# Attention and mixture of experts: VectorE's block of ranks and gates split over two steps, its one-hot tables three to a step, and one filling product at the head

## Chip, cores and metric

The kernel runs on one core of a Trainium2 chip. The metric is the device time of one execution in microseconds (us), the median of several runs. The core has five engines with an instruction queue each: TensorE (matrix products, PE in the rows), VectorE (DVE), ScalarE (ACT), GpSimd (POOL) and SyncE (SP, which issues most transfers). An engine takes its instructions in order and waits on semaphores.

## What is computed

Causal attention over a window of 128 with a distance bias, and then a layer that sends each token to one of eight experts, each of which takes at most `capacity` tokens in the order of their numbers:

```python
scores = scale * np.matmul(q, k.transpose(0, 1, 3, 2))      # (4, 8, 576, 64) each
mask = (rel >= 0) & (rel < window)                           # window = 128
scores = np.where(mask, scores + bias[None], -1000000000.0)
attn = np.exp(scores - scores.max()); attn /= attn.sum() + 1e-09
x = np.matmul(attn, v)                                       # to (2304, 512)
logits = x @ w_gate                                          # 8 experts
expert_idx = np.argmax(logits, axis=1)
# token i goes to slot counts[e] of its expert e while that is below capacity
h = np.maximum(np.einsum('ecd,edf->ecf', disp, w1), 0.0)
y = np.einsum('ecf,efd->ecd', h, w2)
out[i] = gate_w[i] * y[expert_idx[i], pos[i]]                # gate_w: its softmax probability
```

## The kernel before

**Passes and steps.** Four batches are worked in two passes (`batch(0)`, `batch(1)`), two batches in each. A pass has 9 tiles of 128 tokens, and each tile two steps, one for four of the eight heads. So a pass has 18 steps, `kk` 0 to 17; below, "step n" is step n of the second pass. All engines have a function `batch` that runs over the same steps, and semaphores tie them together.

**TensorE in a step:** transposes of the next q tile (even steps) or k tile (odd steps) by `turn` (L1280); of the probabilities of this step (L1322); `turn_back` (L1352), which brings the result of the step before back to token order with its logits, and which waits for `biased`, the count of minima, since it writes the PSUM bank in which the scores of the next step lay; the scores of the step after next (L1314); and `mix` (L1341), probabilities times values, first with the tile's own values and then with `v_step` and the part of the probabilities that GpSimd has masked.

**VectorE in a step:** in odd steps the copy of the turned k (`turned_k`, L930) and the inverse of the sums (`invert_sums`, L936 and L938); `normalise` of the step before (L949, L955, and in even steps the logits' reduce L961); `pick` (L907) and `bias_minimum` (L920) for the step after next; and behind these the work on routing, when it is due.

**ScalarE in a step:** copies out of PSUM and the exponentials of the next step, which wait for the minima. **GpSimd in a step:** `keep_later` (L624), a mask over the probabilities, in odd steps `step_v` (L605), and its share of the routing's tables, `place_in_columns` (L630).

**Routing** is done in three groups of tiles: group 0 is the nine of the first pass, group 1 the next five, group 2 the last four. For group 0 in the steps 1 to 8 and for group 1 in the steps 10 to 17 (in the code `since` counts from the group's first step, 0 and 9) VectorE finds the expert (`find_top`, `find_best`, since 1), its one-hot row (`choose`, since 2), and at since 4 takes the ranks that TensorE has counted and runs `rank_and_weigh`: the gate and, for each token, `key` (its column of slots) and `within` (its place in the column). From these, tables are made: `in_tile` by VectorE (L1023) and `in_column` by GpSimd (L630), one of each for a tile of tokens. TensorE multiplies the two to find out which token fills which slot. For group 0 it does so at step 10 for expert 0's first tile, for the rest behind the steps.

**The head.** TensorE starts with transposes of the identity (`fill_early`, L1457) that nobody reads, and turns the first q and the first k tile between them. Their rows come by four transfers, issued by SyncE (L444) and ScalarE (L801) for half a tile each.

Of the kernel before, what the change touches and what calls it, by code (L numbers as in the profile page):

```python
# [34 lines left out]
def attention_moe(nc, q, k, v, w_gate, w1, w2, capacity, out):  # L35
# [54 lines left out]
    with ctx:  # L90
# [433 lines left out]
        def _(pool):  # L524
# [102 lines left out]
            def place_in_columns(n, lo, hi):  # L627
                pool.wait_ge(keys_ready, n + 1)
                for u in range(lo, hi):
                    g.tensor_scalar(in_column[:, u, :], iota_key[:, :], key[:, u:u + 1], None,  # L630
                                    ALU.is_equal).then_inc(onehots_ready, 1)
# [10 lines left out]
            for b in range(SPANS):  # L642
                for kk in range(STEPS):
                    u = b * TI + kk // 2
                    if kk >= 2:
                        keep_later(b, kk)
                    if b == 1 and kk == FIRST_INVERTED + 1:
                        gather_first()
                    if kk % 2 == 1 and u + 1 < UNITS and (u + 1) % TI > 0:
                        step_v(u + 1)  # L650
                    if 0 <= b * STEPS + kk - 4 < 4 * CHUNKS:
                        split_weights(b * STEPS + kk - 4)
                    if b == 1 and 5 <= kk < FIRST_ROUTED[1]:
                        place_in_columns(0, 2 * (kk - 5), GROUPS[0][1] if kk == 8 else 2 * (kk - 4))
            place_in_columns(1, *GROUPS[1])
            place_in_columns(2, BY_DVE, UNITS)

# [232 lines left out]
        def _(dve):  # L890
# [3 lines left out]
            def link(ins):  # L894

                steps[0] += 1
                ins.then_inc(dve_step, 1)
                dve.wait_ge(dve_step, steps[0])
# [85 lines left out]
            def choose(lo, hi):  # L984

                vec.tensor_tensor(onehot[:, lo:hi, :], by_expert(iota_e[:, :], lo, hi),
                                  by_token(best[:, lo:hi], E), ALU.is_equal).then_inc(onehot_ready, 1)
                vec.tensor_tensor(less_top[:, lo:hi, :], logits[:, lo:hi, :], by_token(top[:, lo:hi], E),
                                  ALU.subtract).then_inc(less_ready, 1)
# [6 lines left out]
                                         .rearrange("p (u e) -> p u e", e=E),  # L996
                                         onehot[:, lo:hi, :], ALU.mult)

            def rank_and_weigh(n, lo, hi):

                if n == 2:
                    own_ranks(n, lo, hi)
                dve.wait_ge(expd_ready, n + 1)
                link(vec.tensor_reduce(gate_sum[:, lo:hi], expd[:, lo:hi, :], AX.X, ALU.add))
                vec.tensor_reduce(rank[:, lo:hi], own_rank[:, lo:hi, :], AX.X, ALU.add)
                link(vec.tensor_scalar(gate_eps[:, lo:hi], gate_sum[:, lo:hi], 1e-9, None, ALU.add))

                vec.tensor_scalar(rounded[:, lo:hi], rank[:, lo:hi], -(P - 1) / 2, ROUND_TO_128, ALU.add, ALU.add)  # L1010
                link(vec.reciprocal(gate[:, lo:hi], gate_eps[:, lo:hi]))
                dve.sem_inc(gate_ready, 1)
                link(vec.tensor_scalar(past[:, lo:hi], rounded[:, lo:hi], ROUND_TO_128, None, ALU.subtract))
                vec.scalar_tensor_tensor(out=key[:, lo:hi], in0=best[:, lo:hi], scalar=float(P * KEEPS),
                                         in1=past[:, lo:hi], op0=ALU.mult, op1=ALU.add)
                link(vec.tensor_tensor(within[:, lo:hi], rank[:, lo:hi], past[:, lo:hi], ALU.subtract))
                dve.sem_inc(keys_ready, 1)

            def place_in_tiles(lo, hi):
                for u in range(lo, hi):  # L1020
                    if EARLY <= u < BY_DVE:
                        vec.tensor_scalar(in_column[:, u, :], iota_key[:, :], key[:, u:u + 1], None, ALU.is_equal)
                    vec.tensor_scalar(in_tile[:, u, :], iota_p[:, :], within[:, u:u + 1], mark[:, u:u + 1],  # L1023
                                      ALU.is_equal, ALU.mult).then_inc(tiles_placed, 1)

            def batch(b, first=False, last=False):
                for kk in range(STEPS):
# [53 lines left out]
                                          cap[:, 0:1], None, ALU.is_lt)  # L1081
                    if last and since == 4:
                        dve.wait_ge(early_kept, 1 if n == 0 else 3)
                        rank_and_weigh(n, lo, hi)
                    if last and n == 1 and since == 5:
                        vec.tensor_copy(is_full_i[:, :], is_full[:, :]).then_inc(is_full_ready, 1)
                    if last and since >= 5:
                        at = lo + (2 * (since - 5) if n == 0 else max(0, 2 * since - 11))
                        place_in_tiles(at, hi if n == 0 and since == 8 else
                                       min(hi, at + (1 if n == 1 and since == 5 else 2)))  # L1090

            vec.memset(v_front[0:HALF, :], 0.0).then_inc(v_front_zeroed, 1)
            link(vec.memset(eps[:, :], 1e-9))
# [32 lines left out]
            find_top(*GROUPS[2])  # L1126
            find_best(*GROUPS[2])
            choose(*GROUPS[2])
            rank_and_weigh(2, *GROUPS[2])
            place_in_tiles(*GROUPS[2])  # L1130

# [142 lines left out]
        def _(pe):  # L1274
# [183 lines left out]

            fill_early(16)
            turn_q(0, 0)  # L1460
            fill_early(4)
            turn_k(0, 0, probsT_ps)
            fill_early(4)
            score(0, 0)
# [191 lines left out]
```

## Time and profile before

| | before |
|---|---|
| time, median of 3 runs (lowest to highest) | 392.94 us (392.62 to 393.62) |
| the profiled execution: its time, its span | 392.7 us, 390.9 us |
| TensorE busy | 375.1 us (96%) |
| VectorE, ScalarE, GpSimd busy | 252.2, 202.0, 144.5 us |
| first pass, second pass, then the experts (from the span's start) | to about 69, 135, 385 us |

The span runs from the first to the last recorded instruction of one execution. "Busy" is time with an instruction under way. TensorE's matmuls overlap, so its share tells little of how near it is to its peak; what costs time are its idle stretches, and what they wait for. In a timeline an instruction's own time is given as well as the idle time ahead of it.

### The profile page before, as it was taken

Reading aid. Unit: us, or ns where it says so; the run is one execution under the profiler, and the core shown is the slowest. Engines: PE = TensorE matmul, PEld = TensorE weight load, DVE = VectorE, ACT = ScalarE, POOL = GpSimd, SP = SyncE. Lnnn points to the kernel's source line nnn. Section 1 sums busy time; section 2 is a strip of 40 time slices with the busy share of each in tenths; the row PEclk is TensorE's granted clock in tenths of the full one; section 3 lists DMA queues with packets and bytes.
Section 4 is the critical chain, followed back from the end, with each engine's and each line's share of the span. In section 5 each row is a group of like instructions: output and inputs, shape, how many; then the busy total and the mean of one; then the engine's idle time right before and its main releaser. Section 6 shows DMA issues by size and latency. Waiting matters only on the chain.

```text
span 390.9 us, 8488 instructions
## 1 busy us (share of the span) xinstructions
PE 375.1 (96%) x2978; PEld 324.2 (83%) x2978; DVE 252.2 (65%) x797; ACT 202.0 (52%) x535; POOL 144.5 (37%) x192
## 2 busy tenths in 40 slices
PE   7999999998999999999999999999999999999990
PEld 7787788786877677989999989889899899989980
DVE  6788677799988673867966546556768674441120
ACT  2978878886887613645634424534646544311100
POOL 7548989935742542232050023034051340020011
PEclk9999999999999999999999999999999999999997
DMA  8999999999751112877685365554787664010001
GB/s 167 201 308 196 231 235 223 263 262 212 169 107 42 43 29 73 268 242 229 200 283 169 119 226 167 179 185 159 238 271 225 195 214 154 3 47 25 2 21 55
DMA packets 81324, 64.87 MB, mean 166 GB/s; under 512 B 63982, under 2 KB 63982, under 8 KB 81264
## 3 DMA queue, kind: packets, MB, share of 16 engines
q1 hardware_dynamic: 73600, 52.19, 49.9%
q0 software_dynamic: 3840, 11.03, 8.6%
q10 hardware_dynamic: 3824, 0.80, 1.1%
q8 instruction: 44, 0.72, 0.8%
q14 instruction: 16, 0.13, 0.1%
HBM read 54.56 MB, written 11.02 MB: 168 GB/s over the span
## 4 chain that ended last, share of the span: by engine, by line
PE 79%; POOL 10%; DVE 5%; issue 2%; ACT 1%; DVEq 0%; POOLq 0%
PE ps L1483 59%; PE ps L1341 4%; PE ps L1314 4%; POOL weights_sb L617 4%; PE ps L1280 3%; PE ps L1352 3%; PE ps L1476 2%; POOL probsT L624 2%; PE ps L1322 2%; POOL v_step L605 2%; POOL weights_sb L616 2%; PE ps L1457 1%; DVE ps L907 1%; DVE probs L920 1%; PE ps L1398 0%
## 5 line engine op out<-in xcount | busy, mean ns | idle before, releaser
L1483 PE MATMUL ps<-rowsT_hi,weights_sb 128*128 128x256 f32 (+2 forms) x512 | 118.2, 309 | 0.9 <-DVE rowsT_lo L1161 0.9
L1483 PE MATMUL ps<-weights_sb,hiddenT 128*128 128x512 f32 x480 | 118.3, 393 | 0.0
L1483 PEld LDWEIGHTS ps<-weights_sb,hiddenT 128*128 128x128 f32 x480 | 88.0, 188 | 16.4 <-DVE hiddenT L1180 0.2
L857 ACT ACTIVATE hiddenT<-ps 128x384 fp32r<-128x384 f32 (+1 forms) x64 | 30.6, 478 | 115.9 <-PE ps L1483 102.6
L1483 PEld LDWEIGHTS ps<-rowsT_hi,weights_sb 128*128 128x128 f32 x512 | 87.0, 188 | 2.5 <-issue 1.4
L1188 DVE TENSOR_TENSOR weights_sb<-raw,weights_sb 128x1024 fp32r<-128x1024 f32 x56 | 68.5, 1223 | 17.7 <-ACT weights_sb L845 15.6
L1483 PE MATMUL ps<-rowsT_lo,weights_sb 128*128 128x256 f32 (+2 forms) x256 | 78.2, 306 | 0.0
L1180 DVE SCALAR_TENSOR_TENSOR hiddenT<-ps,hiddenT 128x384 fp32r<-128x384 f32 (+1 forms) x64 | 34.5, 540 | 59.4 <-ACT hiddenT L857 57.3
L845 ACT ACTIVATE weights_sb<-raw 128x1024 fp32r<-128x1024 f32 x56 | 58.9, 1052 | 0.0
L682 POOL DMA_INDIRECT gathered<-x_rows,src_row x21 | 22.0, 1049 | 92.8 <-DVE weight_now L1174 88.2
L743 ACT ACTIVATE probs<-probs,mins 128x128 f32<-128x128 f32 x144 | 55.7, 393 | 0.4 <-DVE mins L920 0.4
L696 POOL DMA_INDIRECT out<-y_sb,dst_row x21 | 24.4, 1160 | 84.0 <-DVE y_sb L1194 80.3
L1483 PEld LDWEIGHTS ps<-rowsT_lo,weights_sb 128*128 128x128 f32 x256 | 48.2, 188 | 1.2
L624 POOL TENSOR_SCALAR_AFFINE_SELECT probsT<-probsT 128x512 f32<-128x512 f32 x32 | 20.3, 635 | 42.0 <-ACT probsT L769 42.0
L1314 PE MATMUL ps<-kT,qT 64*64 64x192 f32 (+3 forms) x480 | 28.8, 333 | 0.0
L743 ACT ACTIVATION_READ_ACCUMULATOR probs<-probs,mins 128x1 f32 x144 | 27.7, 192 | 0.0
L769 ACT ACTIVATE probsT<-ps 128x512 f32<-128x512 f32 x36 | 21.4, 595 | 10.3 <-PE ps L1322 10.2
L1352 PE MATMUL ps<-eye_wg,mixT 128*128 128x144 f32 x144 | 24.2, 291 | 2.5 <-DVE mins L920 2.5
L949 DVE TENSOR_TENSOR x_sb<-ps,inv_sums 128x256 f32<-128x256 f32 x36 | 15.3, 424 | 15.6 <-PE ps L1352 14.9
L1194 DVE TENSOR_SCALAR y_sb<-ps,weight_now 128x512 f32<-128x512 f32 x23 | 16.1, 747 | 13.9 <-PE ps L1483 13.9
L907 DVE COPY_PREDICATED ps<-later,ps 128x256 f32<-128x256 int32 (+1 forms) x64 | 22.1, 391 | 4.6 <-PE ps L1314 4.5
L1341 PE MATMUL ps<-probsT,v_rows 128*64 128x128 f32 x288 | 23.7, 285 | 0.1
(174 smaller groups left out, 491.6 us busy)
## 6 DMA issues: line engine op xcount, KB each, us to landing
raw<-in_moe_w SPq DMA_DIRECT2D x64, 512.0 KB, 5.1
q_rows<-in_q SPq DMA_DIRECT2D x16, 256.0 KB, 5.9
v_rows<-in_v SPq DMA_DIRECT2D x16, 256.0 KB, 5.7
x_rows<-x_sb SPq DMA_DIRECT2D x16, 256.0 KB, 4.9
k_rows<-in_k SPq DMA_DIRECT2D x14, 256.0 KB, 6.2
k_rows<-in_k ACTq DMA_DIRECT2D x2, 256.0 KB, 6.8
v_rows<-in_v SPq DMA_DIRECT2D x4, 128.0 KB, 5.6
v_front<-in_v SPq DMA_DIRECT2D x4, 128.0 KB, 6.2
```

The costliest lines, as they stand in the source:

```text
L624: g.affine_select(out=probsT[:, 1, :, :], in_=probsT[:, 0, :, :], compare_op=ALU.is_gt, fill=0.0, base=0, pattern=[[0, QUAD], [-1, P]], ch ...
L696: g.indirect_dma_start(out, bass.IndirectOffsetOnAxis(ap=rows[:, i:i + 1], axis=0), y_sb[:, i, :], None, bounds_check=N - 1, oob_is_err=Fa ...
L743: last = nc.scalar.activation(pr, pr, ACT.Exp, bias=mins[:, kk % 2, n:n + 1], scale=-1.0, accum_out=sums[:, i, h:h + 1])
L845: nc.scalar.activation(weights_sb[:, parity(e), 2 * layer, RAW * j:RAW * (j + 1)], raw[:, j, :], ACT.Copy).then_inc(w_hi[layer], 1)
L857: nc.scalar.activation(hiddenT[0][c % RINGED][:, 0:P * size], hiddenT_ps(c, P * size), ACT.Relu).then_inc(hiddenT_hi, 1)
L907: vec.copy_predicated(both[:, :, 2 * P - earlier[i]:2 * P], later[:, own].bitcast(I32).unsqueeze(1).broadcast_to([P, 2, earlier[i]]), both ...
L1180: vec.scalar_tensor_tensor(out=hiddenT[1][c % RINGED][:, 0:P * size], in0=hiddenT_ps(c, P * size), scalar=0.0, in1=hiddenT[0][c % RINGED][ ...
L1188: vec.tensor_tensor(weights_sb[:, parity(e), 2 * layer + 1, part], raw[:, j, :], weights_sb[:, parity(e), 2 * layer, part].bitcast(F32), A ...
L1314: ins = te.matmul(scores_ps(kk % 2, odd)[rows, 2 * P * n + first:2 * P * n + last], qT[part, u % 2, h // 2, rows], keys, start=True, stop= ...
L1341: last = te.matmul(mixT_ps[DH * odd:DH * odd + DH, n, :], left[:, DH * h:DH * h + DH], probsT[:, part, 2 * odd + n, :], start=(part == 0), ...
L1352: last = te.matmul(back_ps(kk % 2)[:, c, :], mixT[:, c, :], eye_wg[:, 2 * quad + c, :], start=True, stop=True)
L1483: ins = te.matmul(dst, left[a], right[c], start=first and n == 0, stop=last and n == 2)
```

## The change

At since 4 VectorE runs only the first half of the block, now `sum_ranks` (the sums of the gate and of the ranks, with `rounded`). The second half, still `rank_and_weigh` (the reciprocal, `past`, `key`, `within`), runs at since 5, behind that step's minima. The tables follow from since 6. For group 0 they are three in each of the steps 6, 7, 8, where two stood in 5, 6, 7 and three in 8, on VectorE and GpSimd alike. For group 1 they are one, two, two in the steps 15, 16, 17, where they stood in 14, 15, 16. Group 2 runs both halves one behind the other as before. At the head one transpose of the identity stands between the first q and the first k tile, not four.

```diff
@@ -650,8 +650,8 @@
                         step_v(u + 1)
                     if 0 <= b * STEPS + kk - 4 < 4 * CHUNKS:
                         split_weights(b * STEPS + kk - 4)
-                    if b == 1 and 5 <= kk < FIRST_ROUTED[1]:
-                        place_in_columns(0, 2 * (kk - 5), GROUPS[0][1] if kk == 8 else 2 * (kk - 4))
+                    if b == 1 and 6 <= kk < FIRST_ROUTED[1]:
+                        place_in_columns(0, 3 * (kk - 6), 3 * (kk - 5))
             place_in_columns(1, *GROUPS[1])
             place_in_columns(2, BY_DVE, UNITS)
 
@@ -996,9 +996,7 @@
                                          .rearrange("p (u e) -> p u e", e=E),
                                          onehot[:, lo:hi, :], ALU.mult)
 
-            def rank_and_weigh(n, lo, hi):
-
-
+            def sum_ranks(n, lo, hi):
 
                 if n == 2:
                     own_ranks(n, lo, hi)
@@ -1008,6 +1006,9 @@
                 link(vec.tensor_scalar(gate_eps[:, lo:hi], gate_sum[:, lo:hi], 1e-9, None, ALU.add))
 
                 vec.tensor_scalar(rounded[:, lo:hi], rank[:, lo:hi], -(P - 1) / 2, ROUND_TO_128, ALU.add, ALU.add)
+
+            def rank_and_weigh(n, lo, hi):
+
                 link(vec.reciprocal(gate[:, lo:hi], gate_eps[:, lo:hi]))
                 dve.sem_inc(gate_ready, 1)
                 link(vec.tensor_scalar(past[:, lo:hi], rounded[:, lo:hi], ROUND_TO_128, None, ALU.subtract))
@@ -1081,13 +1082,15 @@
                                           cap[:, 0:1], None, ALU.is_lt)
                     if last and since == 4:
                         dve.wait_ge(early_kept, 1 if n == 0 else 3)
+                        sum_ranks(n, lo, hi)
+                    if last and since == 5:
                         rank_and_weigh(n, lo, hi)
                     if last and n == 1 and since == 5:
                         vec.tensor_copy(is_full_i[:, :], is_full[:, :]).then_inc(is_full_ready, 1)
-                    if last and since >= 5:
-                        at = lo + (2 * (since - 5) if n == 0 else max(0, 2 * since - 11))
-                        place_in_tiles(at, hi if n == 0 and since == 8 else
-                                       min(hi, at + (1 if n == 1 and since == 5 else 2)))
+                    if last and since >= 6:
+                        each = 3 if n == 0 else 2
+                        at = lo + max(0, each * (since - 6) - (n == 1))
+                        place_in_tiles(at, lo + each * (since - 5) - (n == 1))
 
             vec.memset(v_front[0:HALF, :], 0.0).then_inc(v_front_zeroed, 1)
             link(vec.memset(eps[:, :], 1e-9))
@@ -1126,6 +1129,7 @@
             find_top(*GROUPS[2])
             find_best(*GROUPS[2])
             choose(*GROUPS[2])
+            sum_ranks(2, *GROUPS[2])
             rank_and_weigh(2, *GROUPS[2])
             place_in_tiles(*GROUPS[2])
 
@@ -1458,7 +1462,7 @@
 
             fill_early(16)
             turn_q(0, 0)
-            fill_early(4)
+            fill_early(1)
             turn_k(0, 0, probsT_ps)
             fill_early(4)
             score(0, 0)
```

The same on VectorE's queue, where a row is an instruction or several alike, with the tiles that it writes and reads. In step 4, behind the minima of step 6, there stood before:

```order
L1006 TENSOR_REDUCE gate_sum<-expd 128x9
L1007 TENSOR_REDUCE rank<-own_rank 128x9
L1008 TENSOR_SCALAR gate_eps<-gate_sum 128x9
L1010 TENSOR_SCALAR rounded<-rank 128x9
L1011 RECIPROCAL gate<-gate_eps 128x9
L1013 TENSOR_SCALAR past<-rounded 128x9
L1014 SCALAR_TENSOR_TENSOR key<-best,past 128x9
L1016 TENSOR_TENSOR within<-rank,past 128x9
L930 COPY kT<-ps 128x4x128
L936 TENSOR_TENSOR sums_eps<-sums,eps 128x8
```

The last two rows belong to step 5. At the same place the changed kernel has:

```order
L1004 TENSOR_REDUCE gate_sum<-expd 128x9
L1005 TENSOR_REDUCE rank<-own_rank 128x9
L1006 TENSOR_SCALAR gate_eps<-gate_sum 128x9
L1008 TENSOR_SCALAR rounded<-rank 128x9
L930 COPY kT<-ps 128x4x128
L936 TENSOR_TENSOR sums_eps<-sums,eps 128x8
```

and at the end of its step 5, where two tables (`in_tile`) stood before:

```order
L1012 RECIPROCAL gate<-gate_eps 128x9
L1014 TENSOR_SCALAR past<-rounded 128x9
L1015 SCALAR_TENSOR_TENSOR key<-best,past 128x9
L1017 TENSOR_TENSOR within<-rank,past 128x9
L949 TENSOR_TENSOR x_sb<-ps,inv_sums 128x256
L955 TENSOR_TENSOR gate_part<-ps,inv_sums 128x32
```

Four small instructions have moved behind the minima of step 7, ahead of step 6's `normalise`. For group 1 the block of step 13 stood ahead of the lower half of the first expert tile's rows (`first_rowsT_lo`) and of step 14:

```order
L1010 TENSOR_SCALAR rounded<-rank 128x5
L1011 RECIPROCAL gate<-gate_eps 128x5
L1013 TENSOR_SCALAR past<-rounded 128x5
L1014 SCALAR_TENSOR_TENSOR key<-best,past 128x5
L1016 TENSOR_TENSOR within<-rank,past 128x5
L1038 TENSOR_TENSOR first_rowsT_lo<-ps,first_rowsT_hi 128x512
L949 TENSOR_TENSOR x_sb<-ps,inv_sums 128x256
```

In the changed kernel its second half stands at the end of step 14, with the flag's copy, ahead of the odd step 15:

```order
L1012 RECIPROCAL gate<-gate_eps 128x5
L1014 TENSOR_SCALAR past<-rounded 128x5
L1015 SCALAR_TENSOR_TENSOR key<-best,past 128x5
L1017 TENSOR_TENSOR within<-rank,past 128x5
L1089 CAST is_full_i<-is_full 128x1
L936 TENSOR_TENSOR sums_eps<-sums,eps 128x8
L938 RECIPROCAL inv_sums<-sums_eps 128x8
L949 TENSOR_TENSOR x_sb<-ps,inv_sums 128x256
```

There the flag's copy and one table stood before, and the four are new.

## Rows read from the trace of the kernel before

**Rows 1.** TensorE's waits, all: who waited for whom, us in total, times, longest.

```profile
PE ps L1352 <- DVE mins L920: 2.5, 3, 1.1
```

**Rows 2.** TensorE's timeline, steps 6 to 8: start, us, instructions, [idle before, releaser].

```profile
92.71 0.66 PE L1280 MATMUL ps<-ident,q_rows 128*128 128x128 f32 x4
...
94.92 0.76 PE L1352 MATMUL ps<-eye_wg,mixT 128*128 128x144 f32 x4 [1.11 <-DVE mins L920]
...
97.44 0.66 PE L1280 MATMUL ps<-ident,k_rows 128*128 128x128 f32 x4
...
100.79 0.66 PE L1280 MATMUL ps<-ident,q_rows 128*128 128x128 f32 x4
...
101.72 0.66 PE L1352 MATMUL ps<-eye_wg,mixT 128*128 128x144 f32 x4
102.30 0.88 PE L1314 MATMUL ps<-kT,qT 64*64 64x128 f32 x16
```

**Rows 3.** VectorE's timeline, steps 4 and 5.

```profile
90.58 0.21 DVE L1011 RECIPROCAL gate<-gate_eps 128x9 f32<-128x9 f32 x1
...
91.15 0.59 DVE L1014 SCALAR_TENSOR_TENSOR key<-best,past 128x9 f32<-128x9 f32 x1
...
91.96 0.69 DVE L930 COPY kT<-ps 128x512 f32<-128x512 f32 x1
92.57 0.41 DVE L936 TENSOR_TENSOR sums_eps<-sums,eps 128x8 f32<-128x8 f32 x1
...
93.70 0.75 DVE L907 COPY_PREDICATED ps<-later,ps 128x256 f32<-128x256 int32 x2
...
95.20 0.67 DVE L1023 TENSOR_SCALAR in_tile<-iota_p,within,mark 128x128 f16<-128x128 f16 x2
```

**Rows 4.** GpSimd's timeline, steps 5 and 6.

```profile
91.09 0.63 POOL L624 TENSOR_SCALAR_AFFINE_SELECT probsT<-probsT 128x512 f32<-128x512 f32 x1 [3.40 <-ACT probsT L769]
91.69 1.28 POOL L605 TENSOR_TENSOR v_step<-v_rows 128x512 f32<-128x512 f32 x1
...
94.56 0.63 POOL L624 TENSOR_SCALAR_AFFINE_SELECT probsT<-probsT 128x512 f32<-128x512 f32 x1 [0.33 <-ACT probsT L769]
```

**Rows 5.** Timelines, steps 14 to 17: ScalarE, VectorE, GpSimd, then TensorE.

```profile
123.46 0.60 ACT L786 ACTIVATE first_rowsT_hi<-ps 128x512 fp32r<-128x512 f32 x1 [0.19 <-PE ps L1419]
...
124.91 0.69 DVE L1038 TENSOR_TENSOR first_rowsT_lo<-ps,first_rowsT_hi 128x512 fp32r<-128x512 f32 x1
...
126.25 0.75 DVE L907 COPY_PREDICATED ps<-later,ps 128x256 f32<-128x256 int32 x2
...
128.08 0.15 DVE L936 TENSOR_TENSOR sums_eps<-sums,eps 128x8 f32<-128x8 f32 x1
...
129.08 0.76 DVE L907 COPY_PREDICATED ps<-later,ps 128x256 f32<-128x256 int32 x2
...
127.48 0.64 POOL L624 TENSOR_SCALAR_AFFINE_SELECT probsT<-probsT 128x512 f32<-128x512 f32 x1 [2.22 <-ACT probsT L769]
128.08 1.29 POOL L605 TENSOR_TENSOR v_step<-v_rows 128x512 f32<-128x512 f32 x1
...
127.46 0.76 PE L1352 MATMUL ps<-eye_wg,mixT 128*128 128x144 f32 x4 [0.68 <-DVE mins L920]
...
130.63 0.73 PE L1352 MATMUL ps<-eye_wg,mixT 128*128 128x144 f32 x4
...
132.71 0.66 PE L1322 MATMUL ps<-ident,probs 128*128 128x128 f32 x4
```

**Rows 6.** The head: weight loads (PEld), issue of k rows, issue to landing.

```profile
5.71 0.87 PEld L1457 LDWEIGHTS ps<-ident 128*128 128x128 f32 x4
6.56 0.77 PEld L1280 LDWEIGHTS ps<-ident,k_rows 128*128 128x128 f32 x4
7.29 0.47 PEld L1457 LDWEIGHTS ps<-ident 128*128 128x128 f32 x4
...
1.70 0.82 SPq L444 DMA_DIRECT2D k_rows<-in_k  x1
...
k_rows<-in_k SPq DMA_DIRECT2D x1, 128.0 KB, 4.8
```

## The prediction, made before the changed kernel had run

> **What bounds the kernel now.** I read the list of waits first, for what TensorE waits for. TensorE is busy 96% of the span, and the largest thing its matmuls wait for is VectorE's minima: three times, 2.5 us [rows 1]. Then TensorE's timeline of the second pass over the batches. A step (two per tile of tokens) begins with the four transposes of L1280. Steps 7 to 8 stand 3.35 us apart (97.44 to 100.79) with TensorE never idle, but step 6 took 4.73 us (92.71 to 97.44) [rows 2]. Its L1352, which starts 0.93 us into a free step (100.79 to 101.72), started 2.21 us in, 1.11 us of it idle for VectorE; restart included the step lost 1.38 us. L1352 waits because it writes the PSUM bank whose scores VectorE must have taken for the next step.
>
> Then VectorE's timeline, for why it was late: after the minima of step 6 it ran the block of ranks and gates to the end (the reciprocal of L1011 at 90.58, next step's copy at 91.96) [rows 3]. And GpSimd's beside it, which shows a second thing. VectorE's key (L1014, 128x9) took 0.59 us, where a sum of 128x8 takes 0.15 [rows 5], and ended at 91.74, when GpSimd's L624 ended (91.09 + 0.63). Its tiny sum L936 took 0.41 us and ended at 92.98, when GpSimd's L605 ended (91.69 + 1.28) [rows 3, 4]. The reciprocals, reduces and PSUM readers beside such work show no stretch. So a VectorE instruction with both inputs in SBUF waits until the GpSimd instruction under way is over.
>
> For the second group the picture repeats at step 15: L1352 at 127.46 after 0.68 us idle [rows 5]. The third stall (step 12) follows code that the change leaves alone. After the attention TensorE runs the experts with no wait on a transfer, so a shift of the attention's end should reach the end of the program whole.
>
> **The change part by part.** Of the eight instructions of the block, four now follow the minima of step 4 (13), and four (reciprocal, past, key, within) those of step 5 (14).
>
> *Group 0, the gain.* Step 5 on VectorE starts where the reciprocal stood, 90.6 instead of 91.96. Its copy takes 0.61 (92.57 less 91.96) [rows 3], so L936 comes at 91.2, into L624 of GpSimd, and ends with it at 91.74. From there the old spacing holds (L936's end 92.98 to L907 93.70, 0.7): L907 at 92.44. TensorE could go 1.22 after L907 (94.92 less 93.70), so at 93.66. Step 6 of TensorE starts at 92.71 as before and its L1352 wants 93.64. The stall is all but gone, and step 7 starts near 96.1 (92.71 plus 3.35) instead of 97.44: 1.3 us won.
>
> *Group 0, what is late next.* The four moved instructions start 1.50 after L907 (93.70 to 95.20) [rows 3], at 93.94. Key comes 0.57 later (90.58 to 91.15), at 94.51. GpSimd's L624 of step 6 stands at 94.56, 1.85 after the step's start [rows 2, 4]; both move forward by 0.07 at most, the time for which the step's first transposes had waited for the late copy. It will run from 94.5 to 95.15. Key, or at the latest within behind it, waits for it, and step 6 of VectorE starts at 95.3. Even steps reach L907 0.75 later, as in the other group (124.91 to 126.25, less the 0.60 of L1038 [rows 5]; the logits' reduce is in it): 96.05; the minimum that TensorE wants at 97.27, against 97.03: 0.24 lost, with the restart 0.34. Then three tables of L1023. Two took 0.67 beside GpSimd's columns [rows 3]; three should take 0.7 to 0.9, from 97.55 to 98.25 or 98.45. The copy puts L936 of step 7 at 98.86 or later. GpSimd's L624 of step 7 is 97.95 to 98.58, and behind it comes L605 with 1.28 us, to 99.86. L936 falls into L605 and waits 1.0 us for its end. L907 then stands at 100.55, the minimum at 101.77; step 8 began at 99.8 and wants it at 100.72. TensorE stalls 1.05, starts L1352 at 101.77 and step 9 2.52 later (94.92 to 97.44) [rows 2]: 104.29. The old step 9 began at 100.79 + 3.35 = 104.14. Group 0 in sum: 0.15 us lost.
>
> At this place a page of the skill bears on the sum. The Trainium skill, SBUF — State Buffer, section "SBUF: two separate sides", says that VectorE and GpSimd share a port pair as an exclusive lock held for a whole instruction, also for a VectorE instruction with two SBUF inputs against a GpSimd one that reads SBUF. The trace agrees (0.59 and 0.41 us, both ending with GpSimd's). By the lock the group loses 0.15 us; by free ports it would win 1.3.
>
> *GpSimd's own queue.* Its columns come three to a step from step 6 instead of two from step 5. They wait for the keys, ready at 95.3 now, and should be through by about 97.2, before L624 of step 7. In step 7 the third one puts L624 of step 8 at about 101.7, some 0.1 late, under TensorE's stall. Nil.
>
> *Group 1, the gain.* L1038 stood at 124.91 behind the block. It needs ScalarE's upper half, ready at 124.06 (123.46 + 0.60) [rows 5], so 124.10 now, and L907 at 125.44 instead of 126.25. The minimum is there at 126.65; TensorE's L1352 wanted 126.78 (127.46 less the 0.68 idle). Stall gone, 0.7 won and 0.1 of restart.
>
> *Group 1, what is late next.* The moved four start at 126.94, key at 127.5 (0.57 behind, as in group 0), within just after. GpSimd's L624 starts at 127.48 [rows 5] and does not move, since the transposes ahead of it don't. Within waits to 128.11, and behind it the flag's copy puts L936 near 128.4. In the old kernel L936 came at 128.08, in the very moment in which L605 started, and passed (0.15 us). Now it waits for L605's end at 129.37 (128.08 + 1.29). L907 of step 15 then comes at 130.1 instead of 129.08, the minimum at 131.3. TensorE's L1352 of step 16 started at 130.63 in the old kernel and would now at 131.3: 0.7 late. Behind it the old step waited for GpSimd before its second half (L1352 to the next L1322, 130.63 to 132.71, is 2.08) [rows 5]; that wait is over by then, so the step, which has no scores, needs only 2.52 less their 0.88 [rows 2], 1.65, and ends near 133.0: 0.3 us lost.
>
> *The head.* Three transposes of the identity go, 0.87/4 = 0.22 us each [rows 6], on paper 0.65 us. But the k rows that follow were issued at 1.70 and landed 4.8 later, at 6.5, and TensorE began to load them at 6.56. The fillers merely covered this transfer. The gain lies between 0 and 0.06; I take 0.
>
> *Sum.* 0.15 + 0.3 + 0 = 0.45 us slower: 392.7 of the profiled execution (span 390.9 and 1.8 around it) becomes 393.15. Its own time lies 0.24 under the median of three, 392.94, which would become 393.4. I say 393.3. This kernel's runs spread by 0.3%, 1.2 us, and less can't be told from no change.
>
> **The rivals.** *The two stalls simply go* (faster). For it: the block is plainly what TensorE waited for. Against it: rows 3 and 4, where L936 and key end with GpSimd's instruction. Needed is that key, within and both L936 miss GpSimd's work, or that the lock is no rule. Then group 0 wins 1.3, group 1 some 0.7 (the minimum of step 16 at 130.0, then held by the exponentials), in all about 2.0: 391.0. Chance 0.20.
>
> *One group escapes* (within the noise). Margins are 0 to 0.3 us: key and within at 94.5 to 94.6 against 94.5, L936 at 98.86 against 98.58, key and within at 127.5 to 127.6 against 127.48. If the first or second is off, group 0 wins 1.0 and the sum is -0.7; if the third, group 1 wins 0.6 and the sum is -0.45: 392.3. Chance 0.18.
>
> *The fast clock comes late* (slower). Four transposes took 0.87 us at 5.71 and 0.47 at 7.29 [rows 6]: TensorE went from 1.2 to 2.4 GHz near 7.1, after fillers and q transposes without a break. Now it idles for 0.6 us (5.93 to 6.56) just ahead of that. If the rise comes only after another stretch of work, the k transposes, the first scores and the q transposes run at the low level, three pieces of 0.4 us each (0.87 less 0.47): 1.2 us, and with the 0.45 a time of 394.5. It decides only if it puts the first exponentials back, since they lead on to the GpSimd chain of the first pass. Chance 0.10. The Trainium skill, TensorE: Matmul & The Clock Gate, Part 4, says that transposes don't count as activity for this gate; that would take the risk away, but the trace, whose transposes sped up after nothing but transposes, speaks against it.
>
> **How the numbers follow.** Forecast (both groups caught by GpSimd) 0.50, own range 392.8 to 393.8; both stalls gone 0.20; one escape 0.18; late clock 0.10; the rest 0.02. The range leaves out the farther half of the fast case and most of the slow one: 391.1 to 394.2. Faster by over 0.3% (under 391.8): 0.22. Slower by over 0.3% (over 394.1): 0.09. Between: 0.69.
>
> **What the profile after would show.** Right: TensorE's stall in step 6 nearly gone, a new one of about 1 us in step 8 behind L936 stretched to about 1 us beside L605; none in step 15, but a late L1352 in step 16, with L936 of step 15 stretched likewise; key or within ending with a GpSimd L624; L1280 of the k rows still at 6.5 to 6.6. Wrong: L936 of 0.16 us in steps 7 and 15, step 9 starting near 103.1, or transposes of 0.22 us after 7.5.

## The result, and the profile after

The changed kernel took 394.46 us (median of 5 runs, 394.16 to 395.5) where the kernel before took 392.89 in the same five turns: ratio 1.0039, 95% interval 1.0024 to 1.0054, so 0.9 to 2.1 us slower. Run again later beside its variants it took 393.98 against 393.06 (1.0021, 1.0011 to 1.0031). Forecast were 393.3, so 0.45 us slower by its sum, and a range to 394.2: the sign of the point was right, its size was two to three and a half times too small (0.45 against 0.92 and 1.57), and the range was too short on that side for the first comparison, while the second one's median lies inside it. One execution each of two kernels below, e5 and e7, took 930 and 2049 us; without it their medians would be 390.66 and 393.31 instead of 390.72 and 393.38.

TensorE's waits after, from the list of waits (who waited for whom, us in total, times, longest), which answer to [rows 1]:

```profile
PE ps L1356 <- DVE mins L920: 2.3, 2, 1.4
PE ps L1284 <- DMA k_rows<-in_k: 1.4, 1, 1.4
PE ps L1284 <- DVE kT L930: 0.6, 1, 0.6
PE ps L1345 <- DVE first_slot L1053: 0.5, 1, 0.5
```

The minima cost TensorE nearly what they did, but in other steps: the sum moved from 2.5 to 2.3 us and a wait for VectorE's copy of kT, which the kernel before did not have, stands beside it. TensorE's timeline of steps 6 to 9 after (start, us, in brackets the idle time ahead), for [rows 2]:

```profile
96.54 0.66 PE L1284 MATMUL ps<-ident,k_rows 128*128 128x128 f32 x4
97.75 0.76 PE L1356 MATMUL ps<-eye_wg,mixT 128*128 128x144 f32 x4
...
100.92 0.66 PE L1284 MATMUL ps<-ident,q_rows 128*128 128x128 f32 x4 [0.57 <-DVE kT L930]
...
102.86 0.76 PE L1356 MATMUL ps<-eye_wg,mixT 128*128 128x144 f32 x4 [0.85 <-DVE mins L920]
...
105.38 0.66 PE L1284 MATMUL ps<-ident,k_rows 128*128 128x128 f32 x4
```

Step 7 began at 96.54 instead of 97.44: the old stall is gone, as forecast. Step 9 began at 105.38 instead of 104.14. From step 5 (89.64 here, 89.29 before) to step 9 TensorE took 15.74 us where it took 14.85. VectorE's and then GpSimd's timeline of the same stretch, for [rows 3, 4]:

```profile
94.86 0.64 DVE L1015 SCALAR_TENSOR_TENSOR key<-best,past 128x9 f32<-128x9 f32 x1
...
96.54 0.75 DVE L907 COPY_PREDICATED ps<-later,ps 128x256 f32<-128x256 int32 x2
98.04 2.22 DVE L1024 TENSOR_SCALAR in_tile<-iota_p,within,mark 128x128 f16<-128x128 f16 x3
100.18 0.68 DVE L930 COPY kT<-ps 128x512 f32<-128x512 f32 x1
100.78 0.15 DVE L936 TENSOR_TENSOR sums_eps<-sums,eps 128x8 f32<-128x8 f32 x1
...
94.85 0.63 POOL L624 TENSOR_SCALAR_AFFINE_SELECT probsT<-probsT 128x512 f32<-128x512 f32 x1 [1.52 <-ACT probsT L769]
...
98.34 0.64 POOL L624 TENSOR_SCALAR_AFFINE_SELECT probsT<-probsT 128x512 f32<-128x512 f32 x1 [0.70 <-ACT probsT L769]
98.94 1.27 POOL L605 TENSOR_TENSOR v_step<-v_rows 128x512 f32<-128x512 f32 x1
```

Read them against each other. Key ends at 95.50, when L624 ends (95.48). The three tables were priced at 0.7 to 0.9 us and took 2.22: they end at 100.26, when L605 ends (100.21). So it is not L936 that waits in step 7 (0.15 us) but the tables ahead of it, and the copy of kT, which would have run beside L605, now stands behind it. That makes the new wait of 0.57 us.

Steps 14 to 17, VectorE, GpSimd and TensorE, for [rows 5]:

```profile
128.72 0.60 DVE L1017 TENSOR_TENSOR within<-rank,past 128x5 f32<-128x5 f32 x1
...
129.53 1.03 DVE L936 TENSOR_TENSOR sums_eps<-sums,eps 128x8 f32<-128x8 f32 x1
...
128.65 0.66 POOL L624 TENSOR_SCALAR_AFFINE_SELECT probsT<-probsT 128x512 f32<-128x512 f32 x1 [2.22 <-ACT probsT L769]
129.28 1.26 POOL L605 TENSOR_TENSOR v_step<-v_rows 128x512 f32<-128x512 f32 x1
...
127.29 0.66 PE L1326 MATMUL ps<-ident,probs 128*128 128x128 f32 x4
127.94 0.73 PE L1356 MATMUL ps<-eye_wg,mixT 128*128 128x144 f32 x4
...
132.49 0.76 PE L1356 MATMUL ps<-eye_wg,mixT 128*128 128x144 f32 x4 [1.41 <-DVE mins L920]
...
136.93 0.73 PE L1487 MATMUL ps<-weights_sb,first_rowsT_hi 128*128 128x512 f32 x2
```

This group went as forecast, each row of it: no wait in step 15, within and L936 both end with a GpSimd instruction, and a late L1356 in step 16. From L1326 of step 15 to the first expert product are 9.64 us, 9.32 before (126.12 to 135.44): 0.32 lost, 0.3 forecast.

Two more differences of this trace were no part of the forecast. Step 5 came 0.35 later: at the head the k rows landed 5.5 us after their issue (4.8 before [rows 6]). And in step 10 TensorE waited 0.54 us for first_slot, the last row of the waits above; this is called the hiccup of step 10 below.

### The profile page after: what moved, and what is told of

Read it like the earlier page. It is cut to its first block, busy times and chain, and to the rows that moved or that the text cites. A ratio compares the mean times of both kernels' runs of the same rounds, so it can differ in the third digit from the quotient of the medians.

```text
span 392.4 us, 8482 instructions
## 1 busy us (share of the span) xinstructions
PE 373.7 (95%) x2975; PEld 322.8 (82%) x2975; DVE 254.4 (65%) x797; ACT 202.0 (51%) x535; POOL 144.6 (37%) x192
## 4 chain that ended last, share of the span: by engine, by line
PE 74%; POOL 10%; DVE 8%; issue 2%; DMA 2%; SPq 1%; ACT 0%; DVEq 0%; POOLq 0%
PE ps L1487 59%; POOL weights_sb L617 4%; PE ps L1345 3%; PE ps L1318 3%; PE ps L1356 3%; PE ps L1480 2%; PE ps L1284 2%; POOL v_step L605 2%; POOL probsT L624 2%; DMA v_rows<-in_v 2%; POOL weights_sb L616 2%; DVE ps L907 2%; PE ps L1326 1%; DVE probs L920 1%; SPq L386 1%
## 5 line engine op out<-in xcount | busy, mean ns | idle before, releaser
L624 POOL TENSOR_SCALAR_AFFINE_SELECT probsT<-probsT 128x512 f32<-128x512 f32 x32 | 20.4, 638 | 42.5 <-ACT probsT L769 40.1
L1356 PE MATMUL ps<-eye_wg,mixT 128*128 128x144 f32 x144 | 24.4, 292 | 2.5 <-DVE mins L920 2.3
L949 DVE TENSOR_TENSOR x_sb<-ps,inv_sums 128x256 f32<-128x256 f32 x36 | 15.2, 424 | 14.7 <-PE ps L1356 13.7
```

The costliest lines, as they stand in the source:

```text
L624: g.affine_select(out=probsT[:, 1, :, :], in_=probsT[:, 0, :, :], compare_op=ALU.is_gt, fill=0.0, base=0, pattern=[[0, QUAD], [-1, P]], ch ...
L1356: last = te.matmul(back_ps(kk % 2)[:, c, :], mixT[:, c, :], eye_wg[:, 2 * quad + c, :], start=True, stop=True)
```

## The experiments

Medians below stand beside those of the kernel before on the same chip. Four kernels shared a chip in each of three batches. Unless said otherwise they have four fillers at the head, so that only the split differs.

**The parts alone.** e1 is the kernel before with one filling product:

```diff
-            fill_early(4)
+            fill_early(1)
             turn_k(0, 0, probsT_ps)
```

> The old kernel with one filling transpose at the head instead of four, nothing else. Theory A (the fillers merely covered the transfer of the k rows; they landed 0.7 us later in the profiled execution of the changed kernel by chance): no change of the time, within 0.3 us of the old kernel, and step 0 of the second pass starts within 0.1 us of the old one's. Theory B (the head is a cause of its own: the transfer lands late whenever the fillers are gone, or the clock comes late): 0.35 us slower or more, with the k transposes near 7.3 again. Theory C (the head was the main part of the loss): over 1 us slower.

e2 is the opposite, the whole change with four fillers.

> The changed kernel with four filling transposes again. Theory A: as slow as the changed kernel but for noise, so about 1.2 to 1.6 us over the old one. Theory B: 1.2 us over the old one (1.55 less 0.35). Theory C: within 0.5 us of the old one.

e3 splits group 0's block alone, with three tables a step there, and e4 group 1's alone. The line that does it in e3 (in e4 it has `(False, True)`; the tables' steps, not shown, follow):

```diff
-                    if last and since == 5:
+                    if last and since == (5 if (True, False)[n] else 4):
                         rank_and_weigh(n, lo, hi)
```

> Only group 0 is changed (its block split over the steps 4 and 5, its tables three to a step on VectorE and GpSimd); group 1 and the head as in the old kernel. Theory A (VectorE's third table and L936 wait for GpSimd's mask and v_step): step 9 starts 0.9 us later than in the old kernel, counted from step 5, and the whole is 0.9 us slower; the three tables of step 6 take some 2.2 us again. Rival (the loss of group 0 in the profiled execution was an accident of its phase, 0.35 us late from the head): 0 to 0.3 us slower, tables of step 6 under 1 us.

> Only group 1 is changed (block split over the steps 13 and 14, tables a step later), the rest as in the old kernel. Theory A: the stall of step 15 gone (0.7 us won), a stall of about 1.4 us in step 16 behind L936 stretched to about 1.0 us, in sum 0.3 us slower. Rival (L936 is on no path that matters, the stall of step 16 comes from group 0's lateness): 0.7 us faster, L936 of step 15 undisturbed.

Measured, with before at 393.11: e1 393.42 (1.0008, 0.9994 to 1.0021), e2 394.28 (1.0024, 1.0011 to 1.0037), e3 394.20 (1.0019, 1.0003 to 1.0035), e4 393.63 (1.0016, 1.0003 to 1.0029). Each half of the split costs something by itself and the head nothing that can be told from nothing. The forecasts for e3 met neither side whole: its tables took 1.07 us, not 2.2 and not under 1, and steps 5 to 9 lost 0.30 us, not 0.9, though its median lies 1.09 over before; the hiccup of step 10 is in its trace and in those of e1 and e2. The medians don't divide 1 us further; the traces do. From step 5 to step 9 TensorE took 14.85 us in e1 and e4, as before, and 15.14 and 15.15 in e2 and e3. From step 15 to the first expert product it took 9.32 in e3, as before, and 9.65 in e2 and e4. So group 0 costs 0.30 here, group 1 costs 0.33, and the two add.

Group 0's loss is 0.30 in these, not the changed kernel's 0.89. Both kernels reach the tables equally far behind the start of step 7, 1.50 and 1.49 us. In e2 VectorE, then GpSimd:

```profile
98.09 1.07 DVE L1024 TENSOR_SCALAR in_tile<-iota_p,within,mark 128x128 f16<-128x128 f16 x3
99.08 0.68 DVE L930 COPY kT<-ps 128x512 f32<-128x512 f32 x1
99.69 0.70 DVE L936 TENSOR_TENSOR sums_eps<-sums,eps 128x8 f32<-128x8 f32 x1
...
98.39 0.72 POOL L624 TENSOR_SCALAR_AFFINE_SELECT probsT<-probsT 128x512 f32<-128x512 f32 x1 [0.70 <-ACT probsT L769]
99.09 1.27 POOL L605 TENSOR_TENSOR v_step<-v_rows 128x512 f32<-128x512 f32 x1
```

Here the tables are done when L605 begins, the copy runs beside L605, and L936 waits for its end (100.39 and 100.36). Which way it goes is decided at L624, as the tables one by one show: the second and the third in the changed kernel, then the same two in e2.

```profile
98.27 0.76 DVE L1024 TENSOR_SCALAR in_tile<-iota_p,within,mark 128x128 f16<-128x128 f16 x1
98.94 1.32 DVE L1024 TENSOR_SCALAR in_tile<-iota_p,within,mark 128x128 f16<-128x128 f16 x1
...
98.32 0.31 DVE L1024 TENSOR_SCALAR in_tile<-iota_p,within,mark 128x128 f16<-128x128 f16 x1
98.54 0.63 DVE L1024 TENSOR_SCALAR in_tile<-iota_p,within,mark 128x128 f16<-128x128 f16 x1
```

In the changed kernel the second table waits for the end of L624, and so the third one meets L605. In e2 the second goes ahead, L624 takes 0.72 us instead of 0.64, and only the third waits for L624. To the nanosecond, L624 starts 70 to 72 ns behind the second table's start in the three traces in which that table waits (the changed kernel, e12 and e7), and 78 to 83 ns behind it in the four in which it doesn't (e2, e3, e8, e11). No row shows more of why.

**Taking the suspect away.** e5 leaves L936 out, so that the reciprocal reads the sums (the 1e-9 is not added), and e6 does the same to the kernel before:

```diff
-                vec.tensor_tensor(sums_eps[:, i, :], sums[:, i, :], eps[:, :], ALU.add).then_inc(sum_step, 1)
-                dve.wait_ge(sum_step, b * 2 * TI + 2 * i + 1)
-                vec.reciprocal(inv_sums[:, i, :], sums_eps[:, i, :]).then_inc(sum_step, 1)
+                vec.reciprocal(inv_sums[:, i, :], sums[:, i, :]).then_inc(sum_step, 1)
```

The later waits on `sum_step`, not shown, are lowered to match.

> The change with four fillers back at the head, and the sum of L936 (the sums of the softmax plus 1e-9, two SBUF inputs of 128x8) left out: the reciprocal reads the sums themselves, so the 1e-9 is not added. Theory (VectorE's instructions with two SBUF inputs, and its f16 tables, wait for the GpSimd instruction under way, and the waits of L936 in steps 5, 7 and 15 are what eats the split's gain): VectorE reaches L907 of step 6 some 0.55 us earlier, key of group 0 misses the GpSimd L624 and takes 0.15 to 0.2 us, steps 5 to 9 of TensorE take 13.4 to 13.7 us where they took 15.14 with the four fillers, the late mixing product of step 16 is on time, and the median is 391.3 to 392.3, 2 to 3 us under the same kernel with the sum. Rival 1 (the wait moves on to the reciprocal or the normalising product behind it): these are stretched to the end of L605 instead, steps 5 to 9 still take over 14.8 us, and the median stays at 394.0 or above. Rival 2 (the price is in the tables alone): step 6's three tables still take over 1 us and catch L605, steps 5 to 9 take about 14.6, the median 393.6.

> The kernel before with the sum of L936 left out in the same way (1e-9 not added), its block of ranks and gates undivided. Control for the run without the sum on the changed kernel: how much of that gain is the shorter VectorE queue alone. Theory: the stall of step 6 shrinks from 1.11 to about 0.5 us (0.41 + 0.25 less on VectorE's queue there), those of steps 12 and 15 (0.67 and 0.68) to 0.2 or less, together 1.4 to 1.8 us: median 391.3 to 391.8, and the split kernel without the sum is then not better by more than 0.5 us. Rival (the lock matters only in the split kernel, where L936 falls into L605): the kernel before gains under 0.6 us, median 392.5 to 393.1, and the split kernel without the sum lies at least 0.8 us below it.

Measured, with before at 392.92: e5 390.72 (0.9942, 0.9928 to 0.9956), e6 392.15 (0.9977, 0.9968 to 0.9985). Without L936 the split kernel is 2.2 us faster than before. The theory's numbers for the steps held; the median fell 0.6 us below its range (391.3 to 392.3). TensorE's timeline in e5:

```profile
92.19 0.66 PE L1282 MATMUL ps<-ident,q_rows 128*128 128x128 f32 x4
93.12 0.66 PE L1354 MATMUL ps<-eye_wg,mixT 128*128 128x144 f32 x4
...
98.89 0.66 PE L1282 MATMUL ps<-ident,q_rows 128*128 128x128 f32 x4
99.82 0.66 PE L1354 MATMUL ps<-eye_wg,mixT 128*128 128x144 f32 x4
102.42 0.66 PE L1282 MATMUL ps<-ident,k_rows 128*128 128x128 f32 x4
```

L1354 stands 0.93 behind each step's start, no wait at all, and steps 5 to 9 take 13.58 us. VectorE in the same trace shows why the gain is more than L936's own duration:

```profile
90.73 0.19 DVE L936 RECIPROCAL inv_sums<-sums 128x8 f32<-128x8 f32 x1
...
93.47 0.17 DVE L1013 SCALAR_TENSOR_TENSOR key<-best,past 128x9 f32<-128x9 f32 x1
...
96.18 0.76 DVE L1022 TENSOR_SCALAR in_tile<-iota_p,within,mark 128x128 f16<-128x128 f16 x3
...
97.45 0.19 DVE L936 RECIPROCAL inv_sums<-sums 128x8 f32<-128x8 f32 x1
```

The reciprocal runs in the middle of L624 (GpSimd has it at 90.63 to 91.27) and is not stretched. So VectorE is early enough for key (0.17 us) and for all three tables (0.76) to be through before the next L624. With the wait of L936 in step 5 went those of key and of the tables behind it, and in step 7 there is no L936 to wait. For e6 the forecast was too good (391.3 to 391.8 against 392.15). The stall of step 6 shrank only to 0.65 us: leaving the sum out saves VectorE 0.45 us there (L936 at 92.57, the reciprocal behind it at 93.02 in the kernel before), not the 0.66 that was put in. That of step 15 stayed (0.68): VectorE's last sum before it is that of step 13, behind which VectorE waits 0.56 us for TensorE's scores, with the sum and without it. The rival for e6 was met in part: the split kernel without the sum lies 1.4 below, where it asked for at least 0.8, but the kernel before gained 0.77, where it allowed under 0.6. That 1.4 us is what the split is worth once L936 is gone.

e8 keeps the sum but gives it one SBUF input:

```diff
-                vec.tensor_tensor(sums_eps[:, i, :], sums[:, i, :], eps[:, :], ALU.add).then_inc(sum_step, 1)
+                vec.tensor_scalar(sums_eps[:, i, :], sums[:, i, :], 1e-9, None, ALU.add).then_inc(sum_step, 1)
```

> The change with four fillers back, and the sum of L936 done by a tensor-scalar instruction (one SBUF input and the constant 1e-9) instead of a tensor-tensor one with two SBUF inputs; same values, same place. Theory A (what makes a small VectorE instruction wait for GpSimd is its second SBUF input): L936 takes 0.15 to 0.2 us in steps 5, 7 and 15 where it took 0.56, 0.70 and about 1, and the kernel gains most of what leaving it out gains: steps 5 to 9 take 13.8 to 14.3 us, median 392.3 to 393.0. Theory B (a tensor-scalar instruction from SBUF to SBUF waits as well, as the f16 tables do): L936 keeps its 0.5 to 1 us, steps 5 to 9 take 15.0 us or more, median 394.0 to 394.4.

Measured: 393.36 (1.0008, 0.9997 to 1.0019), steps 5 to 9 15.15 us. VectorE, steps 5, 7 and 15:

```profile
91.01 0.56 DVE L936 TENSOR_SCALAR sums_eps<-sums 128x8 f32<-128x8 f32 x1
...
99.11 0.70 DVE L936 TENSOR_SCALAR sums_eps<-sums 128x8 f32<-128x8 f32 x1
...
128.48 1.04 DVE L936 TENSOR_SCALAR sums_eps<-sums 128x8 f32<-128x8 f32 x1
```

Theory B: it waits as long with one input as with two. My reading that two SBUF inputs make the wait was too narrow. The median lies between the two theories' ranges, 0.4 over before where e2 and e12 lie 1.2 and 1.3 over; the one trace, equal to e2's in these steps, doesn't show why.

**The tables.** e7 gives step 6 two tables, step 7 three and step 8 four. e9 is e7 without the sum, e10 the changed kernel (one filler, three tables) without the sum.

```diff
-                        each = 3 if n == 0 else 2
-                        at = lo + max(0, each * (since - 6) - (n == 1))
-                        place_in_tiles(at, lo + each * (since - 5) - (n == 1))
+                        tables = ({6: (0, 2), 7: (2, 5), 8: (5, 9)}, {6: (0, 1), 7: (1, 3), 8: (3, 5)})[n].get(since)
+                        if tables:
+                            place_in_tiles(lo + tables[0], lo + tables[1])
```

> The change with four fillers back, its group 0 tables on VectorE two, three and four in steps 6, 7 and 8 instead of three in each. Theory (three tables behind the minima of step 6 end just where GpSimd's L605 begins; a third one that is caught costs 0.6 us more than one that passes): the two take 0.5 to 0.7 us, the copy and L936 of step 7 come 0.4 us earlier but L936 waits for the end of L605 all the same, so that steps 5 to 9 take 14.9 to 15.1 us (15.14 with three tables that passed, 15.74 in the changed kernel, whose third was caught), and the median is 393.8 to 394.1, at most 0.4 us under the run with the four fillers and three tables. Rival (the third table, not L936, is what holds step 8 back): steps 5 to 9 take 14.4 us or less and the median is 393.3 to 393.6.

> A try for the best version: four fillers at the head, the block split in both groups, the sum of L936 left out (1e-9 not added) and group 0's tables two, three and four in steps 6 to 8. Theory (with the sum gone, step 6 to 8 already run without a wait behind VectorE: steps 5 to 9 took 13.58 us, four free steps are 13.4): the distribution of the tables is worth 0.2 us at most now, steps 5 to 9 take 13.4 to 13.6, median 390.5 to 391.0, 1.9 to 2.4 us under the kernel before. Rival (two tables instead of three help by themselves, since a caught table costs 0.6 us in part of the executions): 0.3 us or more under the three tables without the sum, which had 390.72.

> The changed kernel itself, with its one filler, without the sum of L936 (1e-9 not added). Beside the same kernel with four fillers and without the sum (390.72) it prices the head alone, in a kernel that has no other stall left to hide a shift. Theory: the k rows' landing sets the head, the fillers only lay beside it: 0 to 0.3 us, median 390.6 to 391.2. Rival (the missing fillers put the whole pass back by the 0.35 us that the changed kernel's trace had at step 5, or the clock rises later): median 391.1 to 391.6, with step 5 of TensorE at 89.2 or later where it was at 88.84.

Measured: e7 393.38 (1.0011, 1.0002 to 1.0020), steps 5 to 9 15.04. The second table was held by L624 this time, so that the two took 0.98 us and not 0.5 to 0.7, and L936 waited for the end of L605 as before. The steps came out as forecast. The median is lower than that and in the rival's range, but equal to e8's with three tables in the same batch, so that it doesn't speak for the rival, whose steps (14.4 or less) did not come. With before at 393.06, e9 took 390.53 (0.9935, 0.9918 to 0.9951), steps 5 to 9 13.57; e10 took 390.60 (0.9945, 0.9927 to 0.9963), steps 13.56. So without the sum the spread of the tables is worth nothing measurable, and e5, e9 and e10 are equally the fastest, 2.2 to 2.5 us under before. e10 lies 0.07 us over e9, of its own batch, and 0.12 under e5, of another, so no price of the head shows in a kernel without another stall to hide it either.

**Kernel or execution?** e11 is the changed kernel again, e12 again the one with four fillers.

> The changed kernel once more, in a batch with its own variants: whether the two things that its first trace had beyond the sum (the third table of step 6 caught by GpSimd's L605, 0.6 us, and a hiccup of 0.5 us at step 10) are of the kernel or of the execution. Theory (both are of the execution: the catch is decided by hundredths of a us, and the hiccup was in four of eight traces, one of them without the split): this trace shows L1024 of step 6 at 1.07 us or 2.22 us and nothing between, and the median is 0.8 to 1.3 us over the kernel before. Rival (both belong to the kernel): 2.22 us and the hiccup again, steps 5 to 9 at 15.7, median 1.4 us or more over before.

> The change with four fillers back, again, in one batch with the changed kernel: the head's price by difference. Theory: 0 to 0.3 us under the changed kernel, 0.6 to 1.1 us over the kernel before; L1024 of step 6 at 1.07 us with L936 of step 7 at 0.70 us, or 2.22 with 0.15. Rival (the head costs 0.5 us or more): 0.5 us or more under the changed kernel.

Measured: e11 393.98 (1.0021, 1.0011 to 1.0031), e12 394.34 (1.0029, 1.0019 to 1.0039). With four fillers the kernel was 0.36 us slower than with one, where 0 to 0.3 faster was forecast, so no price of leaving them out shows. The tables of step 6, VectorE, in e11:

```profile
97.84 1.08 DVE L1024 TENSOR_SCALAR in_tile<-iota_p,within,mark 128x128 f16<-128x128 f16 x3
98.83 0.68 DVE L930 COPY kT<-ps 128x512 f32<-128x512 f32 x1
99.43 0.70 DVE L936 TENSOR_TENSOR sums_eps<-sums,eps 128x8 f32<-128x8 f32 x1
```

and in e12:

```profile
98.48 2.22 DVE L1024 TENSOR_SCALAR in_tile<-iota_p,within,mark 128x128 f16<-128x128 f16 x3
```

The same program showed 2.22 us once and 1.08 once, and so did its neighbour with four fillers (1.07 in e2, 2.22 in e12). Of six traces with the sum and three tables in step 6 two had the long one, nothing lay between, and steps 5 to 9 took 15.1 or 15.7 accordingly. The hiccup of step 10 did not come back in either.

## Why the prediction was wrong

**Both groups caught by GpSimd, so that the split gains nothing:** right. It was the forecast's core, and e5 shows it by taking one wait away. In the first trace it was in step 7 the tables and not L936 that L605 held.

**Group 1, 0.3 lost:** right in each step; 0.32 to 0.33 us in all seven traces in which group 1 is split and the sum is there.

**The head, 0:** right as far as can be told. Step 5 of TensorE began at 89.03 to 89.64 in the four traces with one filler and at 88.84 to 90.08 in the ten with four, 89.39 and 89.43 in the mean. The 0.35 of the first trace was the k rows' landing in that execution. The late clock did not come. The weight loads of the k transposes in the changed kernel took 0.42 us for four, where the low level had taken 0.87 [rows 6]:

```profile
7.28 0.42 PEld L1284 LDWEIGHTS ps<-ident,k_rows 128*128 128x128 f32 x4 [1.59 <-DMA k_rows<-in_k]
```

**Group 0, 0.15 lost:** the step that failed is the price of the three tables, a term that was mis-sized: "Two took 0.67 beside GpSimd's columns [rows 3]; three should take 0.7 to 0.9". The price was read beside L630, next to which the tables run nearly free. But in step 6 they meet L624 and L605, for which they wait, though they have one full input alone. They took 1.07 us, the group then losing 0.30 us, or 2.22, and it lost 0.89. Where they took 1.07, they matter little. In e2 the forecast of the steps 7 and 8 held (8.23 us, 8.19 forecast), since L936 waits for the end of L605 in any case; two tables instead of three (e7) gave back 0.1. The rest of the 0.15 was lost before: TensorE took 6.91 us from step 5 to step 7, 6.81 forecast, because L1356 of step 6 still came late, 1.02 us after the step's start instead of 0.93. Where they took 2.22, step 7 of TensorE took 4.38 us instead of e2's 3.73, the largest part of the miss. I had applied the wait to instructions with two SBUF inputs alone, and did not lay the three tables, 97.55 to 98.45 by my own sum, beside the L624 that I had put at 97.95.

**The sum.** Forecast 0.45. The traces give 0.30 + 0.33 = 0.63 where the third table passes, and 1.22 where it is caught; with two of six caught, about 0.8 (an estimate from few traces). The second comparison's 0.92 agrees. The first's 1.57 is more than even a catch in every execution gives, though its interval begins at 0.9. Of its five executions one has a trace, and it says where the time was in that one: 0.35 at the head, 0.89 in group 0, 0.32 in group 1, and between steps 9 and 15 nothing (21.91 us against 21.98), since step 12, which held one of the three old stalls, gave the hiccup's 0.5 us back: it took 3.70 us instead of 4.28. What the other four executions had is not known. The range's upper end, 394.2, allowed a caught or an escaping group but no second size for the catch.

**Open:** the hiccup of step 10. It stood in four of fourteen traces, the changed kernel's first and e1, e2 and e3, e1 being a kernel without the split. In e1 VectorE took its copy of first_slot (L1052) 1.13 us after it was free, though TensorE's one-column products that it waits for stand at 109.08 to 109.45:

```profile
109.90 0.28 DVE L961 TENSOR_REDUCE logits<-gate_part 128x8 f32<-128x64 f32 x1
111.31 0.16 DVE L1052 COPY first_slot<-ps 128x1 f32<-128x1 f32 x1 [1.13 <-remote]
...
111.52 0.66 PE L1341 MATMUL ps<-probsT,v_rows 128*64 128x128 f32 x8 [1.27 <-DVE first_slot L1052]
```

In the changed kernel's trace the delay stands ahead of another instruction: L949 came 1.27 us behind the start of L1356, and 0.76 in every other trace. No row shows what was late, and no experiment took it away. Both programs that were run a second time, the changed kernel and the one with four fillers, had it once and not the other time, so it belongs to executions and not to the change.

## What to carry to other kernels

Lay each moved small VectorE instruction, those with one input too, beside the GpSimd instruction that runs then, and price it from a row where it met that same GpSimd instruction, not a more tolerant one. Where waits follow on each other, look for the smallest instruction that starts the chain: dropping one sum of 0.15 us took 2.6 to 3.4 us off the split kernel (e8 to e5, e11 to e10), and only then did the moved block pay. If a start lies within 0.1 us of another engine's, give the sum two values and the range both.

## What the runs showed of the hardware

A VectorE tensor-scalar instruction with one full SBUF input, f32 128x8 or f16 128x128 (the tables, which also take two columns as per-partition operands), waits for GpSimd's affine select (L624) and tensor-tensor (L605) as one with two inputs does: 0.56, 0.70 and 1.04 us in e8, 2.22 for three tables. Beside GpSimd's tensor-scalar (L630) two tables took 0.67 [rows 3], against 0.53 alone (at 98.05 in the kernel before), and L936 with its two inputs took 0.15 beside it (at 100.78 in the changed kernel). The reciprocals took 0.17 to 0.21 us and the copies of kT from PSUM 0.67 to 0.69 in all fourteen traces, whatever GpSimd did. The Trainium skill, SBUF — State Buffer, section "SBUF: two separate sides", names the VectorE instructions with two SBUF inputs and those in a 2-port performance mode as holders of the lock; that the first wait is seen here, and if the tensor-scalar ones run in such a mode, theirs is too, but no row shows the mode. The nearly free tables and the free L936 beside L630 don't fit the page's rule, which names GpSimd's instructions without exception. The wait goes both ways: where VectorE's second table went ahead (e2, e3, e8, e11), GpSimd's L624 took 0.72 us instead of 0.64.
